# Attention with decay: the scan's caps and the chunk-end factors on GpSimd instead of VectorE and ScalarE

## The reference

```python
f = 1.0 / (1.0 + np.exp(-f_logit))
for t in range(S):
    state = f[:, :, t, :, None] * state + np.einsum('bhd,bhe->bhde', k[:, :, t], v[:, :, t])
    y[:, :, t] = np.einsum('bhd,bhde->bhe', q[:, :, t], state)
```

## Time and profile before

| | us |
|---|---|
| median of 3 runs | 615.28 (615.19 to 618.15) |
| the profiled execution | 611.62 |
| its span in the profile | 609.7 |
| share of the span that TensorE is busy | 95% |
| VectorE, ScalarE, GpSimd busy | 60%, 48%, 6% |
| mean granted clock of TensorE | 0.991 of full speed |

### The profile page before, as it was taken

How to read it: one execution, slowest core, us unless ns; L and a number is a source line. 1 busy time by engine, 2 the same in 40 slices (tenths; PEclk the granted TensorE clock), 3 DMA queues, 4 the chain that set the end, 5 groups by cost and what they waited for, 6 DMA issues and landing times.

```text
span 609.7 us, 11888 instructions
## 1 busy us (share of the span) xinstructions
PE 577.4 (95%) x4226; PEld 555.4 (91%) x4226; DVE 365.9 (60%) x614; ACT 289.9 (48%) x509; POOL 35.6 (6%) x66
## 2 busy tenths in 40 slices
PE   0899999899998999999999997999999999999997
PEld 0888888899998999999999996999999999989997
DVE  7899999577684458446755575657055704570240
ACT  5799999655564245324623245325222523153112
POOL 3232333000000000000000000000000000000000
PEclk9899999999999999999999998999999999999999
DMA  7879899286101130221033045400130011001102
GB/s 195 207 236 261 257 263 299 68 277 222 32 8 42 71 105 21 73 71 47 13 117 105 29 154 153 133 1 0 53 104 1 0 39 39 0 2 39 40 1 80
DMA packets 31545, 58.74 MB, mean 96 GB/s; under 512 B 3728, under 2 KB 23184, under 8 KB 31504
## 3 DMA queue, kind: packets, MB, share of 16 engines
q1 hardware_dynamic: 31504, 58.21, 31.0%
HBM read 44.04 MB, written 14.16 MB: 95 GB/s over the span
## 4 chain that ended last, share of the span: by engine, by line
PE 65%; DVE 4%; issue 2%; ACT 1%; DMA 1%; DVEq 0%; ACTq 0%; SPq 0%
PE gate_ps L1073 17%; PE ringc L1073 11%; PE small_ps L1073 10%; PE theta_bank L1073 9%; PE mix_ps L1492 6%; PE mix_ps L1497 6%; PE mix_ps L1493 6%; PE mix_ps L1073 2%; PE small_ps L1456 1%; DVE stats L2031 1%; DVE w_lo L78 1%; DMA wc_stage<-in_wC_dram 1%; ACT w_hi L73 0%; DVE z_lo L78 0%; ACT v L1882 0%
## 5 line engine op out<-in xcount | busy, mean ns | idle before, releaser
L1492 PE MATMUL mix_ps<-w_hi,z_hi 128*128 128x384 f32 x288 | 98.8, 343 | 1.0 <-DVE u L1648 0.8
L1493 PE MATMUL mix_ps<-w_lo,z_hi 128*128 128x384 f32 x288 | 96.7, 336 | 0.0
L1497 PE MATMUL mix_ps<-w_hi,z_lo 128*128 128x384 f32 x288 | 73.6, 337 | 0.0
L1073 PE MATMUL gate_ps<-w_hi 128*128 128x384 f32 x192 | 65.2, 340 | 3.9 <-issue 3.9
L1073 PE MATMUL gate_ps<-w_lo,w_hi 128*128 128x384 f32 x192 | 65.1, 339 | 0.0
L1073 PE MATMUL gate_ps<-w_hi,w_lo 128*128 128x384 f32 x192 | 65.0, 339 | 0.0
L1492 PEld LDWEIGHTS mix_ps<-w_hi,z_hi 128*128 128x128 f32 x288 | 54.1, 188 | 1.7 <-DVE u L1648 1.1
L73 ACT ACTIVATE g_hi<-gate 128x384 fp32r<-128x384 f32 x32 | 16.9, 527 | 78.7 <-DVE gate L2081 78.7
L1493 PEld LDWEIGHTS mix_ps<-w_lo,z_hi 128*128 128x128 f32 x288 | 54.2, 188 | 0.0
L2077 DVE TENSOR_TENSOR gate<-gate_ps,b_all 128x384 f32<-128x384 f32 x32 | 17.8, 557 | 59.8 <-PE gate_ps L1073 59.7
L1497 PEld LDWEIGHTS mix_ps<-w_hi,z_lo 128*128 128x128 f32 x288 | 51.8, 188 | 0.4 <-DVE z_lo L78 0.4
(11 more groups left out here) (163 smaller groups left out, 1416.7 us busy)
## 6 DMA issues: line engine op xcount, KB each, us to landing
f_raw<-in_fT_dram SPq DMA_DIRECT2D x32, 144.0 KB, 3.5
k_raw<-in_kT_dram SPq DMA_DIRECT2D x32, 144.0 KB, 3.1
q_raw<-in_qT_dram SPq DMA_DIRECT2D x32, 144.0 KB, 3.5
v_raw<-in_vC_dram SPq DMA_DIRECT2D x16, 288.0 KB, 4.3
xT<-y_sb SPq DMA_DIRECT2D x32, 144.0 KB, 3.5
xt<-xT SPq DMA_DIRECT2D x8, 576.0 KB, 4.1
w_raw<-in_wB_dram SPq DMA_DIRECT2D x6, 768.0 KB, 5.8
u<-xT SPq DMA_DIRECT2D x8, 576.0 KB, 5.1
```

Source lines behind the costliest of these rows:

```text
L1073: done = pe.matmul(out, a, b, start=(first and n == 0), stop=(last and n == len(terms) - 1))
L1492: pe.matmul(out, z, w_hi[:, weights_of[r]], start=(s == 0 and r == 0), stop=False)
L1493: pe.matmul(out, z, w_lo[:, weights_of[r]], start=False, stop=False)
L1497: last = pe.matmul(out, part(z_lo[i], r * DMODEL + d * 128, 128), w_hi[:, weights_of[r]], start=False, stop=(s == ST - 1 and r == 1))
```

## The change

It moves two small steps to GpSimd. `chunk_starts` takes the cap copy out of `sums` and puts it on GpSimd at lag 1, one pipeline step ahead of the scan that uses it. `chunk_ends` goes from ScalarE to GpSimd, and is a plain copy from `w_dn`, which already holds exp(-csum), in place of an exponential of `csum`. The waits are moved along: ScalarE waits for `ends_done` of two pairs back before it writes `w_dn`, in place of before `csum`. GpSimd's list is now `chunk_starts` (1), `sum_tops` (2), `chunk_ends` (2), `mask_scores` (3).

```diff
         @block.gpsimd
+            def chunk_starts(p, b):
+                i = b % 2
+                pool.wait_ge(ln_done.h, ln_done.at(p, 1))
+                if first(p):
+                    pool.wait_ge(cap_set, 2)
+                pool.wait_ge(cs_done.h, cs_done.at(p.back(2), 1))
+                pool.sem_inc(waits_passed, 1)
+                pool.tensor_copy(view(cap[i], 0, [[CHUNK, NCHUNK]]), view(csum[i], 0, [[CHUNK, NCHUNK]]))\
+                    .then_inc(starts_done.h, 1)
+
+            def chunk_ends(p, b):
+
+                i = b % 2
+                if first(p):
+                    pool.wait_ge(rest_cleared, ENDS_CLEARED)
+                pool.wait_ge(w_done.h, w_done.at(p, 1))
+                pool.wait_ge(st_sb.h, st_sb.at(p.back(2), 1))
+                pool.sem_inc(waits_passed, 1)
+                pool.tensor_copy(view(ends[i], 0, [[NCHUNK, HDIM], [1, NCHUNK - 1]]),
+                                 view(w_dn[i], CHUNK - 1, [[0, HDIM], [CHUNK, NCHUNK - 1]])).then_inc(ends_done.h, 1)
...
-            pipeline(pool, [(sum_tops, 2), (mask_scores, 3)])
+            pipeline(pool, [(chunk_starts, 1), (sum_tops, 2), (chunk_ends, 2), (mask_scores, 3)])
...
         @block.scalar
                 act.wait_ge(w_done.h, w_done.at(p.back(2), 2))
-                act.wait_ge(ends_done.h, ends_done.at(p.back(2), 1))
                 act.wait_ge(top_done.h, top_done.at(p.back(2), 1))
...
                 act.wait_ge(q_done.h, q_done.at(p.back(2), 1))
+                act.wait_ge(ends_done.h, ends_done.at(p.back(2), 1))
                 act.activation(w_dn[i][:, :], csum[i][:, :], ACT.Exp, scale=-1.0).then_inc(w_done.h, 1)
-
-            def chunk_ends(p, b):
-
-                if first(p):
-                    act.wait_ge(rest_cleared, ENDS_CLEARED)
-                act.wait_ge(st_sb.h, st_sb.at(p.back(2), 1))
-                act.activation(view(ends[b % 2], 0, [[NCHUNK, HDIM], [1, NCHUNK - 1]]),
-                               view(csum[b % 2], CHUNK - 1, [[0, HDIM], [CHUNK, NCHUNK - 1]]), ACT.Exp, scale=-1.0)\
-                   .then_inc(ends_done.h, 1)
...
         @block.vector
                 if first(p):
                     dve.wait_ge(cap_set, 2)
-                dve.wait_ge(cs_done.h, cs_done.at(p.back(2), 1))
-                dve.tensor_copy(view(cap[i], 0, [[CHUNK, NCHUNK]]), view(csum[i], 0, [[CHUNK, NCHUNK]]))\
-                   .then_inc(starts_done.h, 1)
                 dve.wait_ge(starts_done.h, starts_done.at(p, 1))
                 dve.tensor_tensor_scan(csum[i][:, :], csum[i][:, :], cap[i][:, :], 0.0, ALU.add, ALU.min)\
                    .then_inc(cs_done.h, 1)
```

More of the change, by code:

```diff
@@ L283, in _ @@
         def _(pool):
-            for c in (a_sb, top_done):
+            for c in (a_sb, top_done, starts_done, ends_done):
                 c.open(pool)
@@ L326, in _ @@
             m = mixer["scalar"](act)
-            for c in (a_out, lg_done, ln_done, w_done, ends_done, kt_sb, y_sbd):
+            for c in (a_out, lg_done, ln_done, w_done, kt_sb, y_sbd):
                 c.open(act)
@@ L403, in first_z @@
                     m["first_z"]()
-            pipeline(act, [(neg_logs, 1), (keys_out, 3), (theta_hi, 2), (decays, 2), (growths, 2), (scores_copy, 3), (chunk_ends, 2),
+            pipeline(act, [(neg_logs, 1), (keys_out, 3), (theta_hi, 2), (decays, 2), (growths, 2), (scores_copy, 3),
                            (first_turns, 3), (first_z, 4), (y_out(0), 4), (y_out(1), 4), (first_x, 2)])
@@ L516, in _ @@
             m = mixer["vector"](dve)
-            for c in (f_kept, starts_done, cs_done, q_done, k_done, a_masked, st_sb):
+            for c in (f_kept, cs_done, q_done, k_done, a_masked, st_sb):
                 c.open(dve)
```

## The result

The changed kernel takes 621.04 us (median of 6, 619.08 to 622.42), the kernel before 614.75 (median of 6, the three earlier runs and three beside it). The ratio is 1.0112, with a 95% interval from 1.0087 to 1.0137: about 7 us slower. The profiled executions have spans of 617.3 and 609.7 us.

The account below looks back on a forecast made before the run. VectorE's own line was taken to bound the attention. Ten steady periods +3.8, two last steps +0.7 and first four +0.4 gave +4.9 us: 616.5 profiled, 620.2 for the median, range 614.4 to 623.8.

Parts of the forecast that it names:

- VectorE sets the period, ScalarE's relief is worth nothing: Steady attention: VectorE's own line paces the 5.79 us period; the 0.52 us freed on ScalarE gains nothing by itself.
- The copy arrives under `f_raw`, waits for it and goes ahead of `qs`: GpSimd's ends copy becomes ready during VectorE's `f_raw`, gets in ahead of `qs` and holds it for its own length.
- d: Time the ends copy on GpSimd holds VectorE's `qs` each period: taken as 0.40 us, ends 0.05 and 0.56.
- The select flips to the front of `ks` for 0.32: With `qs` later, GpSimd's first select arrives before `ks` and holds it 0.32 us; period 6.17 with d = 0.40.
- The other branch: If the select did not hold `ks`, both selects behind it would hold the next scan: period 5.71 + 0.02 + d.
- the select takes what the cap copy gave back: Even without d, the period hardly falls below 5.79 us, despite 0.33 us a pair saved on paper on VectorE.
- The cap copy costs nothing on GpSimd: Moved cap copy waits for VectorE's scan to end, then runs beside the score instructions, costing VectorE nothing.
- The ends of the stage: Attention's first four steps add 0.4 us (between 0 and 1.5); the two last, without `f_raw`, add 0.7.
- Rival 1, the relief works: GpSimd's reads never come between VectorE's instructions; attention period falls to 5.46 us, time 611.1; chance 0.14.
- Rival 2: Ends copy slips through, d 0.05 to 0.2: attention period 5.82 to 5.97, time 615.8 to 617.7; chance 0.25.
- Rival 3: GpSimd becomes late: ends copy over 1 us, selects slip; attention period up 0.9 or more, 626 or more; chance 0.08.

Follow-up runs that it names:

- ends_only: Only chunk_ends moved to GpSimd, the cap copy left on VectorE, against the kernel before: 624.34 us, ratio 1.018.
- caps_only: Only the cap copy moved to GpSimd, chunk_ends left on ScalarE, against the kernel before: 611.85 us, ratio 0.9979.
- ends_one_step_later: Changed kernel with chunk_ends one pipeline step later, directly behind chunk_starts in GpSimd's list: 613.78 us, ratio 0.9996 to the kernel before.
- after_no_selects: Changed kernel without its two affine selects a pair (wrong outputs, for timing only): 615.37 us.
- relief_alone: Changed kernel with neither the selects nor the ends copy, GpSimd only signalling in their place (wrong outputs): 613.71 us.
- after: The changed kernel itself, both copies on GpSimd, against the kernel before: 621.04 us, ratio 1.0112.
- packed_read: Changed kernel whose ends copy reads 240 columns side by side in place of a stride of 128 (wrong outputs): 615.93 us.

## Why the prediction was right

- *VectorE sets the period, ScalarE's relief is worth nothing.* Right: ScalarE's waits rose to 4.5 us for the scan alone; `ends_only`, which has the whole of that relief, is the slowest kernel; and `caps_only`, without it, and `ends_one_step_later`, with it, have the same usual period of 5.58.
- *The copy arrives under `f_raw`, waits for it and goes ahead of `qs`.* Right, at 2.79 us behind the scan where 2.78 to 2.87 was expected. That it ends at 57.78 after a start at 56.99, while the free copy takes 0.61, speaks for `f_raw` holding the port; the step of `after_no_selects` in which the copy holds `f_raw` for 0.44 shows it.
- *d between 0.05 and 0.56, taken as 0.40.* It is 0.43. The bound from ScalarE's strided instruction was the better guide (1.8 ns an element against its 2.0), and the packed read gives the low end, 0.19. The Trainium skill's figure (GPSIMD Engine Reference, "Performance pitfalls for Q7 kernels") would have made it an estimated 0.58, too high for the hold that was measured; the copy's whole recorded length, 0.61, is near it. Two slips in the working changed nothing: (292 - 226) / 80 is 0.83, not 0.84, and the lowest d by those numbers is 0.02 (53.95 + 0.20 less 54.13), not 0.05.
- *The select flips to the front of `ks` for 0.32.* Right in the changed kernel. Period 6.17 expected, 6.18 measured. The other branch was off: I had it equal, and with `ks` first the period is 6.00. The error is the point at which the next scan is let in, 5.58 by `caps_only` in place of 5.73. So the sentence that the select takes what the cap copy gave back, even without d, is wrong: without the ends copy 0.2 us a period remain, and it is the flip, which the ends copy brings about, that loses them.
- *The cap copy costs nothing on GpSimd.* Right: it is stretched to the scan's end and touches nobody, and by `caps_only` its move gains 0.2 us a period.
- *The ends of the stage.* Mis-sized: +0.4 for the first four steps and +0.7 for the two last. The span shows +1.95 (1.75 and the first scan's 0.20) and +2.5. I gave each of the last two steps one copy's hold; there the copy waits out `qs` and brings both selects with it ahead of `ks`, 1.35 us in each. A `ks` of 2.29 also stands in the fourth step. How much of the +1.95 is the ends copy's is not shown: in `caps_only`, which has no such copy, the first four periods are already 1.05 longer, and loads and TensorE's scores come late in them. The sum up to the mixer is +8.3 where I had +4.9, and +7.6 over the whole spans; the ratio's interval, 5.3 to 8.4 us, puts 4.9 just outside. That the median came out at 621.04 against 620.2 is luck in part: three more runs put the kernel before 0.5 us lower, and the stretch behind the attention, which I took as the same, was 0.7 us shorter in the profiled execution.
- *Rival 1, the relief works*, falls: `qs` and `ks` are held in every steady step. Even with GpSimd down to its two small copies (`relief_alone`) the mean period was 5.60, not 5.46. *Rival 2*, d below 0.2, would have been the packed read. *Rival 3* did not come: GpSimd was never what TensorE waited for.

## What to carry to other kernels

Before a step goes to an idle GpSimd, list what VectorE does at the moment when it becomes ready: beside instructions with an input in PSUM it was free here; ahead of one with two SBUF inputs it cost VectorE the whole time of its reading. Then look at what its delay flips: an instruction that was second by 0.01 us may come to be first. The order of a list and the lag are the cure, not the number of instructions: the same copy one step later held neither `qs` nor, in most steps, `ks`.

## What the runs showed of the hardware

- Waiting GpSimd instructions are served one after another ahead of VectorE's next one: a copy and two selects held `ks` for 1.35 us in the last step.
- By the hold on `qs`, a read at a stride of 128 columns costs a GpSimd copy 1.8 ns an element (`after`), a packed one 0.8 (`packed_read`).
- GpSimd's hold ends before its recorded end: the next scan was let in about 0.12 us before the select's (`caps_only`).
- The scan takes 1.73 us when its predecessor is VectorE's own state scan, and 1.76 behind the cap copy on which it waits. I have no reason for the 0.03.
- TensorE's clock can fall at the change from attention to mixer. In `relief_alone` the mean granted clock was 0.67 in 112 to 116 us, after four microseconds in which TensorE was busy for only 2.21; the two levels are 2.4 and 1.2 GHz. In the kernel before, with 2.51 of 4 us busy in 108 to 112, it stayed at 1.00:

```profile
108.00:112.00 4.00, 2.21 (x38) 1.00 0.27 74
112.00:116.00 4.00, 4.00 (x39) 0.67 0.00 0
...
108.00:112.00 4.00, 2.51 (x50) 1.00 0.22 60
112.00:116.00 4.00, 3.82 (x43) 1.00 0.06 22
```

  From the last scan to the first mixing product `relief_alone` took 21.25 us and the kernel before 19.44. These 1.8 us are nearly what its ten steady periods had gained. `caps_only` had as little work in 108 to 112 us (2.25 of 4 us) and kept its clock, while `ends_one_step_later` had more (3.44 of 4) and fell to 0.64 in the next four, so what decides stays open.
